# Moving the routing scratch of an RWKV + MoE kernel from its own PSUM bank into the gate bank, on Trainium2

## The reference, cut to what matters

```python
batch, n_heads, seq, head_dim = (4, 8, 768, 48)          # 3072 tokens of 384
g = x @ w_gate                                           # dense layer, d_ff 1536
silu = g * (1.0 / (1.0 + np.exp(-g)))
val = x @ w_val
x = (silu * val @ w_out)
logits = x @ moe2_w_gate                                 # routing, 8 experts
e_idx = np.argmax(logits, axis=1)
eom = 1.0 / (1.0 + np.exp(-(x @ moe2_w_output_gate)))
for e in range(8):                                       # each token through its expert
    h = np.maximum(x[mask] @ w1[e], 0.0)
    ye = h @ w2[e]
    out[mask] = gate_w[mask, None] * eom[mask, e, None] * ye
```

## Time and profile before

| | us |
|---|---|
| median of three runs | 861.91 |
| the profiled execution | 861.91 |
| its span, first to last instruction | 860.1 |
| TensorE matmuls busy | 841.3 (98%) |
| TensorE weight loads busy | 729.8 (85%) |
| VectorE busy | 511.2 (59%) |
| ScalarE busy | 320.2 (37%) |

### The profile page before, as it was taken

How to read it: one execution, slowest core, us unless ns; L and a number is a source line. 1 busy time by engine, 2 the same in 40 slices (tenths; PEclk the granted TensorE clock), 3 DMA queues, 4 the chain that set the end, 5 groups by cost and what they waited for, 6 DMA issues and landing times. The chain is left out here.

```text
span 860.1 us, 19718 instructions
## 1 busy us (share of the span) xinstructions
PE 841.3 (98%) x7827; PEld 729.8 (85%) x7827; DVE 511.2 (59%) x1123; ACT 320.2 (37%) x523; POOL 176.7 (21%) x139
## 2 busy tenths in 40 slices
PE   7999999999999999999999999999999999999995
PEld 5778887778778887788777888899899999999995
DVE  7868545454544354535443444469968877797770
ACT  3423231113111131113111321456467776676651
POOL 2423113222323033203220201004111111111010
PEclk9999999999999999999999999999999999999998
DMA  9443302311113012111200103357987667776700
GB/s 351 143 192 113 113 1 71 103 59 39 58 58 102 22 60 85 58 58 38 79 2 2 38 1 134 162 208 233 394 305 259 242 235 289 288 263 223 266 19 18
DMA packets 23714, 115.70 MB, mean 135 GB/s; under 512 B 3324, under 2 KB 9392, under 8 KB 18016
## 3 DMA queue, kind: packets, MB, share of 16 engines
q1 hardware_dynamic: 19552, 100.14, 32.2%
q0 software_dynamic: 3520, 9.87, 3.0%
q10 hardware_dynamic: 576, 4.72, 1.6%
HBM read 101.63 MB, written 14.16 MB: 135 GB/s over the span
## 5 line engine op out<-in xcount | busy, mean ns | idle before, releaser
L1224 DVE TENSOR_TENSOR PP<-SG,bank 128x512 f32<-128x512 f32 (+1 forms) x78 | 49.9, 646 | 206.2 <-issue 119.4
L1608 PE MATMUL bank<-X1H,WH 128*128 128x512 f32 x432 | 168.5, 391 | 0.3
L1608 PE MATMUL bank<-X1L,WH 128*128 128x512 f32 x432 | 167.9, 390 | 0.2 <-DVE X1L L1047 0.2
L1608 PE MATMUL bank<-X1H,WL 128*128 128x512 f32 x432 | 167.9, 389 | 0.0
L773 ACT ACTIVATE SG<-bank 128x512 f32<-128x512 f32 x72 | 43.0, 597 | 239.6 <-PE bank L1608 237.0
L687 ACT ACTIVATE AH<-PP 128x512 fp32r<-128x512 f32 (+1 forms) x78 | 46.1, 598 | 162.6 <-DVE PP L1224 162.6
L1608 PEld LDWEIGHTS bank<-X1H,WH 128*128 128x128 f32 x432 | 81.0, 188 | 17.9 <-issue 1.3
L1608 PEld LDWEIGHTS bank<-X1H,WL 128*128 128x128 f32 x432 | 81.0, 188 | 17.2 <-DVE WL L1041 0.3
L1608 PEld LDWEIGHTS bank<-X1L,WH 128*128 128x128 f32 x432 | 81.0, 188 | 17.1 <-DVE X1L L1047 0.7
L1227 DVE TENSOR_TENSOR AL<-PP,AH 128x512 fp32r<-128x512 f32 (+1 forms) x78 | 65.2, 842 | 51.0 <-ACT AH L687 51.0
L1655 PE MATMUL bank<-AH,WH 128*128 128x512 f32 (+1 forms) x234 | 92.7, 396 | 0.0
(11 more groups left out here) (223 smaller groups left out, 1800.3 us busy)
## 6 DMA issues: line engine op xcount, KB each, us to landing
W_EVEN<-w SPq DMA_DIRECT2D x20, 1536.0 KB, 8.2
W_ODD<-w SPq DMA_DIRECT2D x18, 1536.0 KB, 8.4
RK_IN<-unit_rk SPq DMA_DIRECT2D x20, 736.0 KB, 4.3
V_IN<-unit_v SPq DMA_DIRECT2D x20, 448.0 KB, 3.4
STG<-w_dense ACTq DMA_DIRECT2D x4, 1152.0 KB, 5.4
XG_ODD<-store SPq DMA_DIRECT2D x9, 394.0 KB, 8.0
store<-PAD SPq DMA_DIRECT2D x8, 394.0 KB
STG<-w_dense SPq DMA_DIRECT2D x2, 1152.0 KB, 8.3
```

The costliest lines, as they stand in the source:

```text
L1224: return tt(PP[:, part], SG[:, part], VALUE_PS[:, part], ALU.mult)
L1608: last = mm(bank_[:, :], lhs[:, f, m, k * P:k * P + P], rhs[:, k, :], start=(x == 0), stop=(x == len(terms) - 1))
```

## The change

For every n but CH, `Routing` lies in bank 0 (`GATE_PS`) instead of bank 7. The routing steps must then not write before ScalarE has read the gate of that f, and the next gate must not be written before VectorE has copied what the step left. The waits on bank 7's other users are gone.

```diff
-            def __init__(self):
-                ps = bank[7]
+            def __init__(self, n):
+                ps = bank[7] if isinstance(n, int) and n == CH else GATE_PS
...
             def route_logits(n):
                 pe.wait_ge(route_loaded, 16)
-                need(pe, ranks_copied, n - 1)
-                logits = Routing().logits
+                logits = Routing(n).logits
...
                     need(pe, silu_ready, q)
+                    if f == (2 if last else 9) and not first:
+                        pe.wait_ge(logits_copied, n)
+                    if f == (3 if last else 10) and not first:
+                        pe.wait_ge(logits_read, n)
+                    if f == (4 if last else 11) and not first:
+                        pe.wait_ge(ranks_copied, n)
                     if f % 2 == 1 and f // 2 < len(units):
                         pe.wait_ge(gate_sums_used, units[f // 2].i + 1 - BATCH)
                     up(GATE_PS, 0, f, n).then_inc(gate_ready, 1)
...
                         if f == (1 if last else 8):
-                            pe.wait_ge(c_used, UNITS if last else units[-1].i + 1)
+                            pe.wait_ge(silu_ready, q + 1)
                             route_logits(n)
                         if f == (2 if last else 9):
+                            pe.wait_ge(silu_ready, q + 1)
                             turn_logits(n)
                         if f == (3 if last else 10):
+                            pe.wait_ge(silu_ready, q + 1)
                             ranks(n)
...
                             pe.wait_ge(silu_ready, q + 1)
-                            if f == 0 and not first:
-                                need(pe, ranks_copied, n - 1)
                             key_sums(u)
...
                         pe.wait_ge(y_added, UNITS)
-                        pe.wait_ge(ranks_copied, CH - 1)
                         turn_rows(EARLY_TILES[0])
```

More of the change, by code:

```diff
@@ L1092, in copy_turned_logits @@
                 dve.wait_ge(logits_turned, n)
-                nc.vector.tensor_copy(LG[:, :, :], Routing().turned.rearrange("p (s e) -> p s e", s=BATCH)[:, :, 0:2 * NE])\
+                nc.vector.tensor_copy(LG[:, :, :], Routing(n).turned.rearrange("p (s e) -> p s e", s=BATCH)[:, :, 0:2 * NE])\
                   .then_inc(logits_read, 1)
@@ L1120, in copy_logits @@
                 dve.wait_ge(logits_ready, n)
-                nc.vector.tensor_copy(LT[:, :], Routing().logits).then_inc(logits_copied, 1)
+                nc.vector.tensor_copy(LT[:, :], Routing(n).logits).then_inc(logits_copied, 1)
             def copy_ranks(n):
                 dve.wait_ge(ranks_ready, n)
-                nc.vector.tensor_copy(RK[:, :, :, :], Routing().ranks).then_inc(ranks_copied, 1)
+                nc.vector.tensor_copy(RK[:, :, :, :], Routing(n).ranks).then_inc(ranks_copied, 1)
             def positions(n):
@@ L1632, in turn_logits @@
                 pe.wait_ge(logits_copied, n)
-                nc.tensor.transpose(Routing().turned, LT[:, :], ident).then_inc(logits_turned, 1)
+                nc.tensor.transpose(Routing(n).turned, LT[:, :], ident).then_inc(logits_turned, 1)
             def ranks(n):
@@ L1637, in ranks @@
                 pe.wait_ge(logits_read, n)
-                placed = Routing().ranks
+                placed = Routing(n).ranks
                 mm(placed[:, 0, :, :], mask, OH[:, :, :], start=True, stop=True)
```

## The result

The changed kernel takes **866.64 us** (median of 5 runs, 865.78 to 867.71) against 861.91 of the kernel before (5 runs, 861.67 to 862.07). The ratio is 1.0058, with a 95% interval of 1.0047 to 1.007: slower by 4.7 us by the medians and 5.0 by the ratio, beyond the 0.2% that a measurement tells from no change. The comparison has fourteen executions of it in all, from 865.66 to 869.05, with the same median. The prediction was 866.2 us, with a range of 865.0 to 867.8. The profiled execution of the changed kernel took 865.66 us, its span is 863.8.

The account below looks back on a forecast made before the run. TensorE bounds the dense stage, so only waits that stall it count: LG 2.95, RK 1.37 and LT 0 make 4.3 us, and 861.9 + 4.3 = 866.2 us, range 865.0 to 867.8.

Parts of the forecast that it names:

- LG: Gate of f = 10, blocks 1 to 5: copy ends 0.37 us late, plus 0.22 restart, 2.95 us together.
- RK: Gate of f = 11: copy 0.01 us late in blocks 1 to 3, 0.12 in 4 and 5; with restarts 1.37 us.
- LT: Gate of f = 9: copy ends 0.48 us before the matmul, 0.25 before its weight load; no cost.
- The restart of 0.22: Extra TensorE delay per binding wait, beyond lateness: release, second semaphore, exposed weight load; 0.22 us, bounds 0.16 and 0.30.
- The nearest row: Gate at block 2, f = 1, waiting for silu_ready and gate_sums_used: stream 0.22 us behind, taken as the restart.
- The sum of 4.3: LG 2.95 plus RK 1.37 plus LT 0 over blocks 1 to 5: 4.3 us; 3.7 to 5.1 with the restart's bounds.
- The removed waits, nothing: Waits on bank 7's other users: c_used and ranks_copied were settled long before, so removing them gains nothing.
- the change of tile shape: Explains the gap before the logits, against the fewer-waits gain of 0.45 us; that rival 3 in 100, with ineffective waits.
- Given back among the experts: Rival: TensorE comes 4.3 us later to the experts and waits 4.3 us less there, 861.9 us; 6 in 100.
- the prediction's own sign of it: Prediction wrong if the distance between the kernels' starts, expected 4.3 us to the end, shrinks among the experts.
- Longer stalls: Rival: restarts cost 0.30 us each and LT's gate loses 0.1 in five blocks, 5.6 us, 867.5; 8 in 100.
- The clock falls: Rival: each of ten dense-stage stalls brings half speed for 4 us, costing 2 us more, 886 us; 2 in 100.

Follow-up runs that it names:

- e2: Changed kernel with only the transposed logits back in bank 7 and the LG wait before the f = 10 gate gone: 863.43 us, ratio 1.0018 to before.
- e7: Changed kernel with one extra 128x128 copy ahead of LT alone: one execution, 871.68 us, with two stretches of half clock.
- e4: Changed kernel with two extra copies ahead of each of the LT, LG and RK copies: 871.92 us, ratio 1.0112 to before.
- e6: On top of e1, own_key (raises gate_sums_used) also moved ahead of the subtraction: 865.96 us against 865.84 for before, ratio 0.9995.
- e5: Changed kernel without the silu_ready wait at the three gates behind routing steps: 869.71 us against 865.84 for before, ratio 1.0042.
- e3: Kernel before, routing in bank 7 and old waits kept, with only the three new copy waits added: 867.07 us, ratio 1.0056.
- e1: Changed kernel with the LT, LG and RK copies moved ahead of VectorE's subtraction: 861.89 us against 861.50 for before, ratio 0.9997.
- e10: The changed kernel, unedited, run again on the third chip: 870.83 us against 866.05 for before, ratio 1.0057.
- e11: The kernel before, unedited, profiled again on the third chip: one execution, 868.41 us.
- e8: Kernel before with the first late tile's rows (XG_ODD) loaded ahead of its second weight matrix W2: 861.95 us against 866.05, ratio 0.9947.
- e9: Changed kernel with the edits of e6 (including those of e1) and e8 together: 860.32 us against 866.05 for before, ratio 0.9936.

## Why the prediction was right, point by point

- **LG, five times 0.37 + 0.22 = 2.95.** Confirmed. The lateness of 0.37 read from before and the restart (0.145 to the gate, 0.08 more to its second matmul) stand in the timeline of after: 0.74 us between starts instead of 0.23, and 0.31 instead of 0.23. That is 0.51 + 0.08 = 0.59 each.
- **RK, 1.37.** Confirmed: 0.38 and 0.49 us instead of 0.23, plus 0.08 each, make 0.23 and 0.34 per site. e2 has this part alone, and its five steps make 1.33 us. The delay at LG does not change the lateness at RK, as the prediction argued.
- **LT, nothing.** Confirmed, for this gate. The reason given was that the weight load had 0.25 us to spare. e7 and e4 make it sharper: it had 0.48 us from the copy's end to the gate, and needs some 0.22 (0.28 was enough in e7, 0.08 cost 0.15 us in e4).
- **The restart of 0.22, with bounds of 0.16 and 0.30.** The nearest row gave the right number: it has the same two semaphores, and from the end of the copy on the ten sites repeat it. But it is not what that wait cost at its own place, as the prediction took it: e6 takes the wait out of the way there and gains 0.10 us, because behind small matmuls part of the weight load is in the open anyway. That it would be the full price behind `down` was not shown by the row, and came true. e5 gives the lower bound, as the earlier trace rows had it for one. The upper bound, with the whole recorded 0.19 us of a weight load exposed, is excluded at all ten sites.
- **The sum of 4.3.** The ten gates lost 4.31 us (2.97 at LG, 1.34 at RK), the dense stage 4.40.
- **The removed waits, nothing.** Confirmed: the first logit matmul comes 0.32 us after its predecessor in all of blocks 1 to 5, in both kernels, though in blocks 2 to 5 it waits for one semaphore fewer now (that the gap comes from the change of tile shape, as the prediction has it, no run shows); and e3, which keeps those waits, costs the same as the change.
- **Given back among the experts.** This rival was wrong in the main, but the prediction's own sign of it does show in the profiled pair: the distance shrinks from 4.41 at 645 us to 3.75 at the end. In e1 it drifts as well (from +0.07 at 645 us to -0.87 at the end) without any dense loss to give back, and in e2, with its loss, it stays at 1.69; so I read it as scatter of the waits for transfers and not as a return.
- **Longer stalls.** Wrong: each of the ten restarts costs 0.22 to 0.23, and the LT gate nothing.
- **The clock falls.** Wrong for this change: ten stalls, 0.35 us of idle time at the longest ones, left the granted clock at 1.00 there, and so did those of 0.75 us in e4. The Trainium skill, "TensorE: Matmul & The Clock Gate", section "A second HAM failure mode: psum-queue depth-cycling", which the prediction names, tells of such swings in another kernel; no run here shows one in the blocks with routing. But the clock does fall in some executions elsewhere, around pauses that are longer than the one the prediction looked at; see the last section.
- **What was missed.** The prediction took the executions of one chip as the spread of the runs. The size of the loss held; the absolute time did not, on two other chips (865.8 and 866.1 us for the kernel before instead of 861.9).

## What to carry to other kernels

When two users are put into one PSUM bank, it is not the sharing that costs but the place of the reader's last instruction: measure from the timeline by how much the copy ends before the matmul that will overwrite it, and if that is under about 0.22 us (measured for a wait on two semaphores in a stream of 128x512 matmuls; 0.16 with one, and less behind small matmuls), count the missing part at each site, once per block. Move the copy to where its engine waits for someone else (here between the product and the subtraction) before taking a bank of its own for it. And read a change's price as a sum over sites, each checked in the trace: the total of 4.7 us is some 0.6% and was still ten stalls that could be pointed at one by one.

## What the runs showed of the hardware that I had not expected

**One load makes most of the difference between two times of the same kernel.** TensorE's pause before the first transposes of XG_ODD was 1.20 to 1.54 us in the traces of before, the change and e1 to e4, where the kernel before takes 861.5 to 861.9 us. In e5, e6, e7, e10 and e11, on the two chips where it takes 865.8 and 866.1, it was 3.43, 3.85, 3.99, 3.84 and 4.48 us. And around each of these longer pauses the granted clock went to 0.50, the 1.2 GHz level, for 3.4 to 6.8 us: in e11 within the pause, in the four others 0.1 to 1.3 us behind its end. The kernel before in e11, by stretch (columns as in rows 1) and the transposes in its timeline:

```profile
616.00:617.00 1.00, 0.00 (x0) 0.00 (x0) 1.00 (x1) 1.00 (x2) 0.00 (x0) 0.93 1.00 397
617.00:623.70 6.70, 4.83 (x17) 4.83 (x18) 5.05 (x7) 4.58 (x5) 0.00 (x0) 0.50 1.01 425
624.00:626.00 2.00, 2.00 (x14) 2.00 (x13) 1.77 (x2) 0.00 (x0) 0.00 (x0) 1.00 1.00 404
...
618.87 0.48 PE L1669 MATMUL bank<-CST,XG_ODD 128*128 128x128 f32 x1 [4.48 <-DMA XG_ODD<-store]
```

Before the fall TensorE had done nothing since 614.4. In the first trace of the same kernel the same stretch is busy at 1.00, and in e8 too; here are before and then e8:

```profile
617.00:623.70 6.70, 6.70 (x41) 6.70 (x40) 5.55 (x7) 3.69 (x5) 2.00 (x1) 1.00 1.01 419
```

```profile
616.00:624.00 8.00, 8.00 (x53) 8.00 (x52) 7.53 (x13) 6.35 (x9) 2.00 (x1) 1.00 1.02 427
```

At 0.50 the matmuls of 128x384 start 0.32 us apart instead of 0.17. The account of e11 against the first trace of before, in starts of TensorE: +0.4 us at 25 us, +1.3 at 29 behind a first stretch of 0.50 from 26.4 to 29.8, still +1.3 at 611, +4.56 at the transposes, that is 3.3 by the longer pause, +6.77 at 628, that is 2.2 by the half clock; 6.5 at the end, which is the distance of the two executions (868.41 against 861.91). The longer pause has two parts. XG_ODD was issued at 610.80, 2.3 us later than in the first trace, of which 1.3 is the lateness of the whole program and 1.0 is new: before the rows the queue waited 5.8 us for the padding stores, where in the first trace it waited 2.1 us for them and 2.7 for the rows' address. And the transfer itself took longer, 8.1 us from the issue to the first reader against 5.8, with the DMA engines' share at 1.0 in both. The queue's wait for the padding, by the view of its waits, in e11 and then in the first trace of before:

```profile
SPq L559 <- DMA store<-PAD: 5.8, 1, 5.8
```

```profile
SPq L559 <- DMA store<-PAD: 2.1, 1, 2.1
```

This wait was 1.5 to 3.2 us in the traces of before, the change and e1 to e4, and 5.0 to 5.8 in those of e5 to e11.

This lies behind the dense stage and bears on both kernels alike, which fits the ratio of the change, 1.0058 and 1.0057 on chips whose times are 4 us apart. It also accounts for a reordering of one load in e8 being worth 4.6 us, where the first trace of before had a pause of 1.2: on that chip the pause and the half clock behind it together cost 5.5 us in e11 beyond what they cost there (e11 is an execution 2.4 us above the median of its chip, and its half clock lasted 6.8 us where that of the other four lasted 3.4). Where the pause is 1.2 us long, the trace would promise about 1 us; that was not measured.

**A pause of 2 us can go either way.** At 25 us TensorE waits before `state_terms` of the first block. 0.3 to 1.7 us of pause there left the clock at 1.00 in all traces; after 2.0 (e7, e11) and 2.8 us (e10) it was 0.50 from about 26 to 30 us, but after 2.0 us in e9 it stayed at 1.00. What decides that, and why padding and rows take longer on two of the three chips, is open; no run here was made for it. Each chip was used at one time only, so the runs do not tell the chip from the moment.
